# Attention and Fourier stage issued in another order: both transforms of a batch with k-v products and the next group between them, two sets of folded tokens

## What is computed

```python
def _attn_ref(q, k, v, g_norm):
    kv = np.einsum('bhsd,bhse->bhde', k, v)
    out = np.einsum('bhsd,bhde->bhse', q, kv)
    rms = np.sqrt(np.mean(out * out, axis=-1, keepdims=True) + 1e-06)
    return out / rms * g_norm

def _moe_ref(x, w_ch1, w_ch2):
    X = np.fft.fft(np.fft.fft(x, axis=1), axis=2)
    u = x + np.real(X)
    un = (u - mean(u)) / np.sqrt(var(u) + 1e-06)      # over the features
    return u + np.maximum(un @ w_ch1, 0.0) @ w_ch2

def _moe2_ref(x, U, V, w_ch1, w_ch2):
    u = x + (x.transpose(0, 2, 1) @ U @ V).transpose(0, 2, 1)
    return u + np.maximum(u @ w_ch1, 0.0) @ w_ch2
```

## Time and profile before

| what | us |
|---|---|
| median of 3 runs | 1757.25 (1756.53 to 1758.02) |
| the profiled execution | 1755.45 |
| its span in the trace | 1753.6 |
| TensorE busy in the span | 1699.4 (97%) |
| VectorE busy | 1377.0 (79%) |
| ScalarE busy | 805.9 (46%) |
| GpSimd busy | 237.1 (14%) |
| last transform over tokens in a whole step (batch 6) starts | 197.85 |
| first large matmul starts | 235.15 |

### The profile page before, as it was taken

The page is one execution under the profiler, slowest core; times in us unless marked ns, Lnnn a source line. Parts: engine busy times, 40 slices in busy tenths (PEclk is TensorE's granted clock), DMA queues, the critical chain, the costliest instruction groups (busy, mean ns, idle before and its releaser), DMA issues.

```text
span 1753.6 us, 27424 instructions
## 1 busy us (share of the span) xinstructions
PE 1699.4 (97%) x10712; PEld 1645.8 (94%) x10712; DVE 1377.0 (79%) x1734; ACT 805.9 (46%) x1169; POOL 237.1 (14%) x171
## 2 busy tenths in 40 slices
PE   6999999899999999999999999999999999999999
PEld 5877789889999999999999999999999999999999
DVE  4999988988888887987976867956857758658567
ACT  1444555545445445445445445435434444443343
POOL 0474340020020020020110110100100100100200
PEclk8999999999999999999999999999999999999999
DMA  7677569998898898898886777966867767767663
GB/s 239 237 246 232 203 230 354 373 356 299 315 336 304 325 318 302 323 315 315 321 283 248 282 228 265 348 229 241 277 222 254 264 229 255 265 221 254 229 248 124
DMA packets 124321, 478.15 MB, mean 273 GB/s; under 512 B 13089, under 2 KB 47201, under 8 KB 83618
## 3 DMA queue, kind: packets, MB, share of 16 engines
q1 hardware_dynamic: 121762, 475.22, 77.3%
q10 hardware_dynamic: 2432, 1.18, 0.3%
HBM read 396.14 MB, written 78.64 MB: 271 GB/s over the span
## 4 chain that ended last, share of the span: by engine, by line
PE 75%; DVE 17%; issue 4%; ACT 1%; DMA 1%; SPq 1%; POOL 1%; DVEq 0%; ACTq 0%
PE pair L958 11%; PE pair L960 11%; PE pair L959 11%; PE pair L989 6%; PE pair L991 6%; PE pair L990 6%; PE pair L978 5%; PE pair L981 5%; PE pair L980 5%; DVE t_lo L1610 3%; DVE t_raw L1629 2%; PE pair L736 2%; DVE w_sb L1538 1%; PE tr_ps L846 1%; PE pair L757 1%
## 5 line engine op out<-in xcount | busy, mean ns | idle before, releaser
L958 PE MATMUL pair<-t_hi,w_sb 128*128 128x384 f32 x1344 | 461.4, 343 | 10.8 <-DVE h_sb L1647 7.2
L959 PE MATMUL pair<-t_lo,w_sb 128*128 128x384 f32 x1344 | 455.9, 339 | 0.0
L960 PE MATMUL pair<-t_hi,w_sb 128*128 128x384 f32 x1344 | 455.6, 339 | 0.0
L1291 ACT ACTIVATE t_hi<-t_raw 128x768 fp32r<-128x768 f32 x240 | 203.1, 847 | 280.0 <-DVE t_raw L1629 279.9
L1610 DVE TENSOR_TENSOR t_lo<-t_raw,t_hi 128x768 fp32r<-128x768 f32 x300 | 302.9, 1015 | 17.7 <-ACT t_hi L1279 16.4
L1856 POOL TENSOR_TENSOR t_raw<-a_sb 128x768 f32<-128x768 f32 x60 | 138.6, 2313 | 1267.0 <-PE pair L981 553.0
L978 PE MATMUL pair<-w_sb,t_hi 128*128 128x256 f32 x1008 | 285.4, 283 | 8.5 <-DVE t_lo L1610 7.9
L980 PE MATMUL pair<-w_sb,t_hi 128*128 128x256 f32 x1008 | 282.6, 280 | 0.0
L981 PE MATMUL pair<-w_sb,t_lo 128*128 128x256 f32 x1008 | 282.5, 280 | 0.0
L958 PEld LDWEIGHTS pair<-t_hi,w_sb 128*128 128x128 f32 x1344 | 252.8, 188 | 19.4 <-issue 14.9
L959 PEld LDWEIGHTS pair<-t_lo,w_sb 128*128 128x128 f32 x1344 | 253.0, 188 | 2.6
(11 more groups left out here) (187 smaller groups left out, 2218.7 us busy)
## 6 DMA issues: line engine op xcount, KB each, us to landing
w_sb<-wc SPq DMA_DIRECT2D x263, 1024.0 KB, 5.4
wc<-w_sb SPq DMA_DIRECT2D x25, 1024.0 KB, 6.3
w_raw<-wr1a SPq DMA_DIRECT2D x24, 512.0 KB, 6.6
w_raw<-wr1b SPq DMA_DIRECT2D x24, 512.0 KB, 4.0
w_raw<-wr2a SPq DMA_DIRECT2D x10, 1024.0 KB, 7.7
wc<-pb_v SPq DMA_DIRECT2D x16, 640.0 KB, 7.0
u_dram<-x_sb SPq DMA_DIRECT2D x24, 384.0 KB, 5.5
res_sb<-u_dram SPq DMA_DIRECT2D x36, 256.0 KB, 7.4
```

The source lines that it names most:

```text
L958: nc.tensor.matmul(ps, w_hi, hi[:, x, :], start=(fresh and x == 0), stop=False, skip_group_check=True)
L959: nc.tensor.matmul(ps, w_hi, lo[:, x, :], start=False, stop=False, skip_group_check=True)
L960: last = nc.tensor.matmul(ps, w_lo, hi[:, x, :], start=False, stop=(x == 1), skip_group_check=True)
L1291: nc.scalar.activation(t_hi[r][:, :, :], t_raw[r][:, :, :], ACT.Copy).then_inc(hi_ready, 1)
```

## The change

- **Two sets of folded tokens.** `ce_sb` and `so_sb` get a second buffer; batch b uses number b % 2. `fold_features(b)` now waits only for the transform of batch b - 2.
- **TensorE.** Step b is now: `attention(b, (1, 2))`, `seq_transform(b - 1)`, `kv_products(b + 1)`, tile 0 of `feature_transform(b - 1)`, `attention(b + 1, (0,))`, tiles 1 and 2. Ahead of step 1 stand all three groups of batch 0, `kv_products(1)` and `attention(1, (0,))`.
- **VectorE.** The product with g_norm is a function of its own (`weigh`), and all three of a batch come after the scaling of groups 1 and 2. `fix_row(b - 2)` comes after them instead of `fix_row(b - 1)` at the end of the step. `sums(b + 1, 0)` and `normalise(b + 1, 0)` lie between the three unfolds.
- **ScalarE.** Both roots (groups 1 and 2) stand ahead of the four `copy_seq`; `square(b + 1, 0)` and `root(b + 1, 0)` lie between the `copy_cos`.
- **The end.** The parts of the last token transform run in a new order without the transposes between them, the transposes follow; `ln_apply` goes from ScalarE to VectorE (`tensor_scalar`), the sum of slot 1 goes from GpSimd to VectorE, `raw(0, 0)` on GpSimd now follows all adds of batch 6, and the two late chunks 4 and 5 are loaded before the store of batch 5.
- **Transfers.** k and v of batch 0 come in two halves by token tiles and a rest, in rows of 4 KB, and the products of batch 0 run by token tile. `flat` merges the two free dimensions of an access; k and v of batch 2 are loaded ahead of the feature constants, k and v of batch b + 2 after q of batch b + 1; a batch is stored in the order of groups 1, 2, 0. The constants have three semaphores instead of one.

```diff
+    folds_at = (a0 + 81248, a0 + 32768)
+    ce_sb = [at(f"ce_sb{r}", o, [PT + 1, NT, LC]) for r, o in enumerate(folds_at)]
+    so_sb = [at(f"so_sb{r}", o + 3104, [PT, NT, LC - 2]) for r, o in enumerate(folds_at)]
...
+            for t in range(2):
+                sp.dma_start(flat(k_sb[0][:, 2 * t:2 * t + 2, :]), flat(k_main[0][:, 2 * t:2 * t + 2, :])).then_inc(kv0_loaded[t], 16)
+            sp.dma_start(k_sb[0][0:64, 4, :], k_rest[0]).then_inc(kv0_loaded[2], 16)
+            sp.dma_start(flat(q_sb[0][:, :, :]), flat(q_t[0])).then_inc(q0_loaded, 16)
...
             def store_u(b):
-                for g in range(NT):
+                for g in (1, 2, 0):
                     if g == 0:
                         sp.wait_ge(row_fixed, b + 1)
...
             def fold_features(b, g, first):
                 dve.wait_ge(eo_ready, 2 * (NT * b + g + 1))
-                if not first:
-                    dve.wait_ge(seq_done, 8 * (b - 1) + 5)
+                if b >= 2:
+                    dve.wait_ge(seq_done, 8 * (b - 2) + 5)
...
+            def ln_apply(q):
+                dve.wait_ge(ln_shifted, 1)
+                u = in_buffer(q)
+                nc.vector.tensor_scalar(u[:, :], u[:, :], ln_ri[:, q:q + 1], ln_shift[:, q:q + 1],
+                                        ALU.mult, ALU.add).then_inc(in_ready, 1)
...
-            for t in range(NT):
-                unfold(B - 1, t, False)
-                if t == 0:
-                    split_slot_lo(1)
+            unfold(B - 1, 0, False)
+            lo_up(0, 0)
+            lo_up(0, 1)
+            split_slot_lo(1)
+            unfold(B - 1, 1, False)
+            unfold(B - 1, 2, False)
...
-                if b == B - 1:
-                    sum_slot(1)
-                for t in range(NT if b < B - 1 else 1):
+                for t in range(NT):
                     add_transform(b - 1, t)
             raw(0, 0)
-            add_transform(B - 2, 1)
-            add_transform(B - 2, 2)
```

More of the change, by code:

```diff
@@ L1196, in phase1_step @@
                 if not more:
                     ln_total(4)
-                copy_seq(b - 1, (3,))
-                if not more:
                     ln_total(5)
                 copy_g(b - 1)
-                copy_row(b)
-                if not more:
+                if more:
+                    copy_kv(b + 1)
+                else:
                     ln_centre(slice(4, 6), 1)
                     ln_square(4)
+                copy_cos(b - 1, 0, first)
+                if more:
+                    square(b + 1, 0, False)
+                else:
@@ L1541, in phase1_step @@
             def phase1_step(b, first, more):
[L1542 removed]
                 sums(b, 1)
[L1544 removed]
+                sums(b, 2)
                 normalise(b, 1)
+                normalise(b, 2)
+                for g in range(NT):
+                    weigh(b, g)
+                if not first:
+                    fix_row(b - 2)
                 fold(b, 0, False)
[L1547 to L1550 removed]
+                fold(b, 1, False)
                 if more:
[L1552 removed]
+                    fold_tokens(b, 2, False)
                     unfold(b - 1, 0, first)
[L1554 removed]
+                    sums(b + 1, 0)
                     unfold(b - 1, 1, first)
[L1556 removed]
+                    normalise(b + 1, 0)
+                    unfold(b - 1, 2, first)
+                    fold_features(b, 2, False)
+                    for n in SUMMED.get(b, ()):
+                        split_unit_lo(UNITS[n])
                 else:
[L1558 removed]
                     fold(b, 2, False)
@@ L1561, in phase1_step @@
                     unfold(b - 1, 1, first)
-                unfold(b - 1, 2, first)
-                fix_row(b - 1)
-                for n in SUMMED.get(b, ()):
-                    split_unit_lo(UNITS[n])
-            sums(0, 0)
-            normalise(0, 0)
-            sums(0, 1)
-            normalise(0, 1)
+                    ln_scale()
+                    for q in range(NCH):
+                        ln_apply(q)
+                    unfold(b - 1, 2, first)
+                    sum_slot(1)
+                    fix_row(b - 1)
+            for g in range(NT):
+                sums(0, g)
+                normalise(0, g)
+                weigh(0, g)
             fold(0, 0, True)
-            sums(0, 2)
-            normalise(0, 2)
+            sums(1, 0)
+            normalise(1, 0)
             fold(0, 1, True)
```

222 lines of the change are left out of this document (100 added, 122 removed).

## The result

The changed kernel takes 1751.86 us in the median of nine runs (1746.86 to 1753.73); the kernel before, run beside it nine times, takes 1757.25. The ratio of the two is 0.9961 with a 95% interval of 0.9945 to 0.9977. Run once more with the experiments it took 1753.51 us (twelve runs), ratio 0.9968 (0.9951 to 0.9985). So it is faster by 0.3 to 0.4%, some 5 us, where 9.0 were forecast. It lies inside the range.

A forecast was written before the change was run, and what follows sets the result against it. VectorE was the slower loop, with TensorE waiting for it. Terms 43.0 + 150.2 + 36.5 put the second large matmul step at 229.7 instead of 238.69, 9.0 us less: median 1757.25 to 1748.2 us, range 1741.5 to 1754.5.

The forecast's parts named there:

- TensorE's 24.2: In a whole step: the time TensorE needs without waits, 24.2 us, where the kernel before takes 26.09.
- the wait for the root's sake: In the steps: TensorE waits at the transform's third slot, roots preceding slot copies; 1.1 us four times, 0.3 twice.
- A to B: Six steps, from the first token transform (A) to the last whole step's (B): 150.2 us, bounds 146.5 to 153.
- (b): Rival, 18%: VectorE stays the bound with its stretching, ln_apply alternates with GpSimd's adds; 4.6 us less, 1752.7 us.
- (c): Rival, 5%: slower, a scaling waits in five steps for the store of group 0 from its buffer; 1764 us.
- (d): Rival, 9%: half the gain, root waits grow to about 1.7 us a step, clock costs 3 us early; 1755.5 us.
- Start to A: From the start to the first token transform: 43.0 us instead of 45.60, bounds 41.3 and 45.
- clock ahead of A: Before the first token transform: TensorE's pauses of about 3 and 2.6 us lower the clock, costing 1.5 us.
- Rival (a): Chance 18%: clock stays up before the first token transform (41.5) and the split hides; 15.4 us less, 1741.9 us.
- B to C: Last whole step's token transform to the large matmuls' second step (C): 36.5 us instead of 40.84, bounds 33.5 and 38.5.
- The rule: VectorE and GpSimd share SBUF ports: at the end, six moved tensor_scalar would each wait behind an add of 0.73 us.
- C to the end: From the second step of the large matmuls to the end: unchanged at 1514.9 us.

The follow-up runs named there:

- r6_roots: Changed kernel with ScalarE copying token transform slots 0 and 1 each ahead of one of the two roots: 1748.50 us, ratio 0.9959.
- r1_same: The changed kernel run again unchanged, for a second trace: 1753.51 us, ratio 0.9968.
- r9_end2: r5_end, but raw(0,2) and raw(0,3) wait until VectorE has split slot 1, and unfold(7,1) goes ahead of that split: 1746.79 us, ratio 0.9928.
- r3_gpsimd_waits: Changed kernel with only a wait for batch 6's fixed row put before GpSimd's three raw sums: 1749.25 us, ratio 0.9954.
- r12_best: r9_end2 with ScalarE's order of r6_roots and ScalarE's high parts of raw(0,2) and raw(0,3) later: 1745.08 us, ratio 0.9941.
- r10_start2: Changed kernel with products of zeros in TensorE's early pauses and batch 2's k and v loaded behind feature matrices and first weights: 1751.54 us, ratio 0.9955.
- r2_row_first: Changed kernel with fix_row(6) on VectorE directly behind the six ln_apply, ahead of the unfold and slot sum: 1749.76 us, ratio 0.9956.
- r11_ln_back: Changed kernel with the six ln_apply back on ScalarE: 1756.65 us, ratio 0.9991.
- r5_end: r2_row_first with raw(0,0) ahead of the adds of (6,2), and raw(0,2), raw(0,3) after VectorE's first two splits: 1750.21 us, ratio 0.9968.

## Why the prediction was right or wrong

**Direction, range and mechanism of the steps: right.** Faster by more than 0.2%, inside 1741.5 to 1754.5. TensorE's 24.2 is 24.15 (`r6_roots`), the fold waits are gone, VectorE's busy time in a step fell from 25.11 to 23.3 us, and the wait for the root's sake is where it was put. In detail the waits are 0.83 four times rather than 1.1, and 0.16 once rather than 0.3 twice, 3.5 us instead of 5.0; VectorE waits for a square (1.23 to 1.68 us) and for no root. That A to B, forecast at 150.2, came out at 149.92 is in part luck: the waits were 1.5 us smaller, and half clock behind A, which the sum did not have, put 1.6 back.

Of the rivals (b), that VectorE stays the bound, falls for the steps: they lost their waits when only ScalarE's order was changed. By its date alone it would have passed: it has C at 234.1, and `r1_same` has 234.40, from other terms (43.38, 149.92 and 41.10 for 43.5, 152.5 and 38.1). (c) did not occur, VectorE waits for no store. (d) falls too: the waits at the roots did not grow to 1.7 us.

**Start to A: near in size, incomplete in cause.** 43.0 was forecast, 43.38 and 43.57 came (42.90 to 44.91 in the ten traces with this start). Two terms failed in opposite directions. The transfers were costed at nothing. The products start at 6.96 instead of 6.2 and end 0.2 to 1.0 us late, and sseq lands so late that in six of the ten traces with the changed kernel's order of transfers TensorE waits 1.1 to 3.5 us for it. The sum looked at bytes and at what covers the first transfers, not at what the issue of the last one in the queue waits for. The other term, clock ahead of A, was right in kind (3.48 and 3.13 us for 1.87) and cost less, since VectorE sets A too. What was forecast nowhere is the loss behind A: pieces of 3.26 and 3.10 us, some 3.2 us in the first trace (27.19 for the step from A, 23.98 in `r9_end2`), and none in `r3_gpsimd_waits`, `r9_end2` and `r12_best`. Rival (a) had the clock stay up and A at 41.5; `r10_start2`, with the clock up and the transfer there, has it at 42.27.

**B to C: wrong, and this is where the gain went.** 36.5 (33.5 to 38.5) was forecast, 41.1 and 42.2 came. VectorE's queue was dated well: `fix_row(6)` starts 25.8 us behind B, inside the forecast's 24.2 to 28.9 for its end, and the `ln_apply` take 4.9 us in all, 0.83 each beside GpSimd's adds. The step that failed is the size of that row fix, taken at its usual 0.7 us. It takes 8.3. The trace of before had shown more, just where GpSimd's `raw` of 1.81 us starts:

```profile
226.53 2.02 DVE L1489 TENSOR_TENSOR x_sb<-mrow_sb,nyq_sb 1x255 f32<-1x255 f32 x1
```

That is the second add of `fix_row(6)`, 2.02 us instead of 0.41. The sum had named every part: that the copy of the first feature tile needs the row, that GpSimd's sums begin at about 28 behind B (28.3), and the earlier trace rows held a split that took 3.71 us beside GpSimd. The rule was applied to the instructions that were moved, and not to the one that thereby came to lie beside GpSimd's longest instructions. `r2_row_first` and `r3_gpsimd_waits` show it: with the row short, TensorE's wait of 6.7 us is gone. It is not all of the loss, since C then came 2.2 to 4.4 us sooner and not 5: low halves took the row's place beside the sums. `r11_ln_back` shows that the moved instructions were worth about 3 us. The number stayed in the range because the 4.6 to 5.7 us that were lost here are less than the 6.3 us from the forecast to its upper end, which had been set there for (b): for this term that is luck.

The Trainium skill (SBUF — State Buffer, Who interferes with whom) has whichever of two such instructions issues first hold the shared ports for its whole length, while the other is blocked. By that rule the row add would have waited for one add or one sum, 1.8 us at most. The trace differs: it was held for 6.33 us from 222.40, through the adds and, by thirds of the 5.49 us, two of the three sums. The split of `r5_end` was held across both of its sums (5.28). Elsewhere the wait is one instruction, as the page has it: the second row add (2.01), a low half in `r2_row_first` (1.68), two adds in `r9_end2` (1.62 and 2.05). The split of 3.71 us in the earlier trace rows too began 0.8 us ahead of two sums and ended at 237.88, ahead of their end at 239.56. The measurement decides: the price lies between one of GpSimd's instructions and several in a row, and which it will be no run explains.

**C to the end: nearly unchanged.** 1513.0 and 1512.2 instead of 1514.9. The kernel before had one wait more there, 0.57 us at 250.09 for VectorE, which came 1.5 us later to its reads; C to D is 0.9 us longer in it. The rest lies behind D, where the traces spread: from D to the end all fourteen have 1487.8 to 1491.4.

The sum of misses: with 149.92 and a B to C of 36.5 `r1_same` would have ended 4.6 us sooner, 11.6 us under the profiled execution of before. Single runs of one kernel spread over up to 14 us, so 0.2% is seen only in medians of ten or so.

## What to carry to other kernels

Before an instruction is moved, look at which instructions thereby become neighbours in time on VectorE and GpSimd, and price those at one of GpSimd's instructions at least and, as the worst case, at several of them in a row, however small they are. Where the trace at hand has such a pair, take its duration there and not the usual one. A one-row fix that other engines wait for belongs ahead of such a run, and the run itself behind the last VectorE instruction on the path. A transfer's date is set not by its bytes alone but by when its queue accepts it and by what is on its way beside it: moving one ahead of another moved a landing by over ten microseconds here.
